# Routing spread over three heads, and five smaller moves, in a fused attention and two-layer mixture-of-experts kernel

## The reference

```python
def _attn_ref(q, k, v):                       # batch 4, 8 heads, 1152 rows, 64 wide
    q_pool = q.reshape(B, H, S // 2, 2, D).mean(axis=3)
    scores = scale * np.matmul(q_pool, k.transpose(0, 1, 3, 2))
    scores = scores - np.max(scores, axis=-1, keepdims=True)
    attn = np.exp(scores)
    attn = attn / (np.sum(attn, axis=-1, keepdims=True) + 1e-09)
    return np.matmul(attn, v).astype(np.float32)
...
x = np.ascontiguousarray(attn_out.transpose(0, 2, 1, 3)).reshape(B * S, H * D)   # 2304 x 512
x = _moe_ref(x=x, **moe_kwargs)     # rows with x @ w_skip > 0: best of 8 experts by x @ w_gate,
                                    # x + gate * relu(x @ w1[e]) @ w2[e]; other rows pass through
return _moe2_ref(x=x, **moe2_kwargs)  # every row: gate * sigmoid(x @ w_output_gate)[e] * relu(x @ w1[e]) @ w2[e]
```

## Time and profile before

| | |
|---|---|
| three timed executions | 1203.83, 1208.31, 1208.90 us (median 1208.31) |
| profiled execution | 1202.06 us, of which the span of the trace is 1200.3 us |
| TensorE busy | 1136.9 us (95% of the span) |
| VectorE busy | 771.9 us (64%) |
| ScalarE busy | 543.3 us (45%) |
| GpSimd busy | 436.1 us (36%) |
| DMA | 132.61 MB, mean 110 GB/s |
| by stage | attention to about 616 us, first expert layer to about 867 us, second to the end |

### The profile page before, as it was taken

The page is one execution under the profiler, slowest core; times in us unless marked ns, Lnnn a source line. Parts: engine busy times, 40 slices in busy tenths (PEclk is TensorE's granted clock), DMA queues, the critical chain, the costliest instruction groups (busy, mean ns, idle before and its releaser), DMA issues.

```text
span 1200.3 us, 22144 instructions
## 1 busy us (share of the span) xinstructions
PE 1136.9 (95%) x7821; PEld 934.8 (78%) x7821; DVE 771.9 (64%) x1710; ACT 543.3 (45%) x945; POOL 436.1 (36%) x335
## 2 busy tenths in 40 slices
PE   7999999999999999999977999999979999999996
PEld 5767767677677776776756999999869999999995
DVE  6667677776787766877462777766745564565551
ACT  3555555555555555555422444544324334334320
POOL 0766666576656775567750000000000000100000
PEclk9999999999999999999988999999979999999999
DMA  5262222232222322222147801454864454151100
GB/s 123 62 208 67 63 70 60 69 93 67 69 61 70 96 73 63 59 69 57 44 173 253 317 27 41 162 199 162 299 216 175 179 183 167 42 178 35 35 18 14
DMA packets 74398, 132.61 MB, mean 110 GB/s; under 512 B 11040, under 2 KB 29472, under 8 KB 74320
## 3 DMA queue, kind: packets, MB, share of 16 engines
q10 hardware_dynamic: 26240, 69.22, 15.7%
q1 hardware_dynamic: 43424, 50.58, 15.6%
q0 software_dynamic: 4656, 11.79, 3.0%
HBM read 106.12 MB, written 19.24 MB: 104 GB/s over the span
## 4 chain that ended last, share of the span: by engine, by line
PE 77%; DVE 16%; DMA 2%; POOL 1%; issue 1%; ACTq 0%; ACT 0%; SPq 0%; POOLq 0%; DVEq 0%
PE PS L723 22%; PE PS L573 8%; PE PS L489 7%; DVE mx L1020 7%; PE PS L556 6%; PE PS L736 6%; PE PS L543 6%; PE PS L737 6%; PE PS L740 6%; PE PS L557 4%; DVE arena_a L994 3%; DVE KA L1003 2%; DVE KA L1000 2%; PE PS L586 1%; PE PS L610 1%
## 5 line engine op out<-in xcount | busy, mean ns | idle before, releaser
L441 POOL TENSOR_TENSOR arena_a<-arena_a,arena_p 128x576 f32<-128x576 f32 x224 | 327.0, 1460 | 143.4 <-ACT arena_p L839 127.7
L1020 DVE TENSOR_REDUCE mx<-PS 128x1 f32<-128x384 f32 (+1 forms) x480 | 249.6, 552 | 156.9 <-PE PS L543 151.4
L723 PE MATMUL PS<-moe,W 128*128 128x128 f32 x2432 | 281.0, 277 | 2.3 <-ACT moe L922 2.3
L723 PEld LDWEIGHTS PS<-moe,W 128*128 128x128 f32 x2432 | 278.1, 193 | 4.7 <-ACT moe L922 2.9
L839 ACT ACTIVATE arena_p<-PS 128x576 f32<-128x576 f32 x288 | 187.6, 652 | 149.9 <-PE PS L557 144.8
L556 PE MATMUL PS<-QHT,KA 128*128 128x288 f32 x576 | 198.6, 348 | 0.5 <-ACT QLT L850 0.5
L543 PE MATMUL PS<-KA,QHT 128*128 128x384 f32 (+1 forms) x480 | 171.8, 359 | 10.3 <-DVE mx L1020 9.6
L1124 DVE TENSOR_TENSOR W2L<-W2R,W2H 128x1024 fp32r<-128x1024 f32 x148 | 175.1, 1245 | 5.0 <-ACT W2H L811 5.0
L557 PE MATMUL PS<-QLT,KB 65*128 65x288 f32 x576 | 169.3, 297 | 0.0
L811 ACT CAST W2H<-W2R 128x1024 fp32r<-128x1024 f32 x148 | 144.3, 1048 | 46.6 <-PE PS L740 41.1
L573 PE MATMUL PS<-arena_p,arena_a 128*64 128x288 f32 x1152 | 160.5, 414 | 1.1 <-issue 1.1
(11 more groups left out here) (173 smaller groups left out, 1211.4 us busy)
## 6 DMA issues: line engine op xcount, KB each, us to landing
W<-in_moe_w ACTq DMA_DIRECT2D x16, 2048.0 KB, 14.4
W2R<-in_moe_w ACTq DMA_DIRECT2D x16, 2048.0 KB
moe<-xs SPq DMA_DIRECT2D x40, 258.0 KB, 4.3
arena_a<-in_k SPq DMA_DIRECT2D x32, 288.0 KB, 2.9
arena_a<-in_v SPq DMA_DIRECT2D x32, 288.0 KB, 2.7
KB<-KA SPq DMA_DIRECT2D x32, 288.0 KB
arena_a<-in_q SPq DMA_DIRECT2D x32, 256.0 KB, 3.2
xs<-padrow SPq DMA_DIRECT2D x8, 258.0 KB, 4.0
```

The costliest lines, as they stand in the source:

```text
L441: nc.gpsimd.tensor_tensor(Acc[u], Acc[u], P[u][:, t, :], ALU.add).then_inc(acc_step, 1)
L723: last = nc.tensor.matmul(PS[:, HB + f // 4, (f % 4) * PN:(f % 4 + 1) * PN], W1[s][:, d, f * PN:(f + 1) * PN], xT[:, d, :], start=(d == 0) ...
L1020: vec.reduce_max(mx3[0:n, t, c:c + 1], PS[0:n, MXB + b % 2, 0:KB_], AX.X).then_inc(pr_max, 1)
```

## The change

Six things are moved; no arithmetic is added or removed.

1. The routing steps of a batch stand in three heads instead of two (`RT_GAPS`); its ranks, exponentials and scatters come one head later.
2. The third of the three block matmuls of t = 4 (`prior` of block 10) stands behind `weighted` and `sums`, no longer ahead of them.
3. `trans_k(g, 1)` waits for the first low part only (`3 * g + 1`).
4. `back_sums` stands behind the last block matmul and directly ahead of `back_logits`, no longer between the two halves of t = 6.
5. The first expert's w2 is split in heads 3 to 6, one chunk each, no longer in head 31. The loads of later weights follow: w2 of expert 2 at the end of head 8, w1 of expert 2 behind the first expert's tiles, and w1 and w2 of expert 10 behind the start of the second layer.
6. In `tile_route` the rank, `Racc` and `Raccb` stand ahead of the wait for `os_free` and the copy to `os_`.

```diff
-        RT_GAPS = {(0, 5): range(4), (0, 10): range(4, 8), (1, 5): range(10, 14), (1, 10): range(14, 18)}
-        SCATTER_IN = {at + 2 + n: (b, range(2 * n, 2 * n + 2)) for b, at in enumerate(RANKS_IN) for n in range(TB // 2)}
+        RT_GAPS = {(0, 5): [0], (0, 10): [1, 2, 3], (0, NBLK): [4, 5], (1, 5): [6], (1, 10): [7], (1, NBLK): [8, 9],
+                   (2, 5): [10, 11], (2, 10): [12, 13, 14, 15], (2, NBLK): [16, 17]}
+        SCATTER_IN = {at + 3 + n: (b, range(2 * n, 2 * n + 2)) for b, at in enumerate(RANKS_IN) for n in range(TB // 2)}
...
+        SPLIT_IN = [3, 4, 5, 6]
...
-                    pe.wait_ge(k_lo, 3 * g + 2)
+                    pe.wait_ge(k_lo, 3 * g + 1)
...
-                    if t == 6 and before:
-                        back_sums(h - 1)
...
                     if t == 4:
-                        if after:
-                            prior(h + 1, next(blocks))
                         if before:
                             weighted(h - 1, 2)
                             sums(h - 1)
+                        if after:
+                            prior(h + 1, next(blocks))
...
-                    if t == 6 and h in RANKS_IN:
-                        ranks_of_batch(RANKS_IN.index(h))
+                    if t == 6 and h - 1 in RANKS_IN:
+                        ranks_of_batch(RANKS_IN.index(h - 1))
                     if t == 6 and before:
+                        back_sums(h - 1)
                         back_logits(h - 1)
...
-                    if h == NH - 1 and 1 <= t <= WCH:
+                    if h in SPLIT_IN and t == 4:
                         act.wait_ge(w2_in[0], 16)
-                        w2_high(0, 0, [t - 1])
+                        w2_high(0, 0, [SPLIT_IN.index(h)])
...
+                if h == SPLIT_IN[-1] + 2:
+                    act.wait_ge(w_lo[0], 1)
+                    load_w2(2)
...
                 if m == 0:
                     act.wait_ge(out_done, NH)
-                    act.wait_ge(w_lo[0], 1)
-                    load_w2(2)
-                    load_w1(2)
+                else:
+                    load_w2(E + 2)
+                    load_w1(E + 2)
...
+                    if w == 0:
+                        load_w1(2)
                     if w + 3 < 2 * E:
                         act.wait_ge(w_lo[m], end + 1)
-                        load_w2(w + 3)
                         act.wait_ge(h_done[m], end * 2)
-                        load_w1(w + 3)
+                        if e < E - 1:
+                            load_w2(w + 3)
+                            load_w1(w + 3)
...
+                    if h in SPLIT_IN and b == 10:
+                        w2_low(0, 0, 0, [SPLIT_IN.index(h)])
+                    route_in(b)
                 if has(h + 1):
                     negate_max(h + 1)
-                if h == NH - 1:
-                    w2_low(0, 0, 0)
                 if has(h - 1):
                     divide(h - 1)
-                if first is not None:
-                    route_step(first, 8)
-                    route_step(first, 9)
+                route_in(NBLK)
...
-                dve.wait_ge(os_free, i + 1)
-                vec.tensor_copy(os_, ob).then_inc(os_done, 1)
                 dve.wait_ge(t_rank, i + 1)
                 then_wait(vec.tensor_tensor(tx[:, :], PS[:, RKB, 0:NR], regbase[:, :], ALU.add))
                 then_wait(vec.tensor_tensor_reduce(out=tx[:, :], in0=tx[:, :], in1=tR[:, :], scale=1.0, scalar=0.0,
                                                    op0=ALU.mult, op1=ALU.add, accum_out=tpf[:, 0:1]))
+                then_wait(vec.tensor_tensor(Racc[:, :], Racc[:, :], tR[:, :], ALU.add))
+                vec.tensor_copy(Raccb[:, :], Racc[:, :]).then_inc(rt_acc, 1)
+                dve.wait_ge(os_free, i + 1)
+                vec.tensor_copy(os_, ob).then_inc(os_done, 1)
                 dve.wait_ge(os_done, i + 1)
                 vec.tensor_tensor(tpu[:, :], tpf[:, :], tinv[:, :], ALU.add).then_inc(t_pos, 1)
-                then_wait(vec.tensor_tensor(Racc[:, :], Racc[:, :], tR[:, :], ALU.add))
-                vec.tensor_copy(Raccb[:, :], Racc[:, :]).then_inc(rt_acc, 1)
```

17 lines of the change are left out of this document (8 added, 9 removed).

## The result

| | before | after |
|---|---|---|
| timed executions, median | 1206.07 us (4 runs, 1201.98 to 1208.90) | 1184.38 us (4 runs, 1183.79 to 1186.12) |
| span of the profiled execution | 1200.3 us | 1182.0 us |
| TensorE busy | 1136.9 us | 1129.2 us |
| VectorE busy | 771.9 us | 759.1 us |

The changed kernel is 1.8% faster: ratio 0.9823, 95% interval 0.9803 to 0.9844. I had predicted 1189 (1178 to 1202).

A forecast was written before the change was run, and what follows sets the result against it. TensorE, busy 95% of the span, was taken as the bound. Terms -9 - 11.2 - 0.4 + 4 - 2.4 - 6.3 - 2.3 + 8 = -19.6 us from 1208.31 gave 1189; range 1178 to 1202, the forecast's own 1182 to 1197.

The forecast's parts named there:

- Ordinary heads: Attention heads: edits 2 and 4 directly save 0.3 us in 30 heads (-9), earlier query pooling 0.40 in 28 (-11.2).
- The earlier pooling: VectorE's query pooling, early in a head: GpSimd's last addition ends about 0.40 us earlier through edit 4, -11.2 over 28 heads.
- The new wait at block 12: After block 10's move, block 12 needs its maximum: late by 0.09 us plus 0.10 for weights not loaded ahead.
- Ninth key tile: Its 0.28 us wait does not come off, as the fifth block waits anyway: 0 in ordinary heads, -0.4 in the first.
- w2's chunks: Heads 3 to 6, behind block 10's maximum: each chunk costs 1.0 us at block 13's matmul, +4 in all.
- Head 31: Split gone from there: value products begin earlier and, no longer the additions, bound the row sums: -2.4 us.
- Loads: Layer starts: row tile arrives early, -6.3 us; loads behind first tile cost 0; second layer's start 0, bound +2.
- Tile routing: Between the layers, edit 6: the count no longer waits for a scatter, net -2.3 us, bounds 0 and -4.
- Routing: Edit 1, routing steps in three heads: 4.0 us per batch against 1.3, so +2.7 each, +8 in all.
- each may wait for an addition: Head ends: steps 4 and 5, likewise 16 and 17, may each wait for GpSimd; next max and pooling some 1.4 us late.

The follow-up runs named there:

- experiment six: Changed kernel with each w1 load one expert later, so two loads, not three, queue behind the first tile and one at the second layer's start: 1183.70 us, ratio 0.9833.
- experiments four: The kernel before with only edits 2 and 4 applied: 1200.37 us, ratio 0.9942.
- seven: Changed kernel with edit 1 alone taken back, routing steps in two heads at their old places: 1199.22 us, ratio 0.9957.

## Why the prediction was right, and where its steps were not

The time came out 4.6 us below the forecast, inside its own range, and the main mechanism, the gain in the ordinary heads, was as I described it. Of the 4.6 us, 2.2 lie in the kernel before: the forecast starts from its median over three runs, 1208.31, and with the fourth run that is 1206.07. That the rest is so small is luck. By the traces the gain is 18.3 us where I had 19.6, but routing cost 7.4 us less than forecast, while the loads (2.6 and 1.6) and the tile routing (3.2) brought 7.4 less.

- **Ordinary heads** (predicted 20.2 us, two terms): 0.65 per head; over 30 heads 19.5. Edit 2 alone is worth 0.45 (predicted 0.17 to 0.3), edit 4 alone 0.32 (predicted 0.40 + 0.10); each is measured with the other in place, and together they make 0.65. The earlier pooling is shown: 0.30 of edit 4's gain stand ahead of the fifth block. The new wait at block 12 is there and in size: 0.16 us of loss where I had 0.19. What I mis-sized is the gain against it, 0.48 behind block 9 where I had 0.36, and I overlooked that edit 2 also makes GpSimd's additions end earlier, for another 0.12 ahead of the fifth block.
- **Ninth key tile** (0): right.
- **w2's chunks** (4.0): 3.3, at block 13 as predicted, right in place and nearly in size. But this is the price of the place that I took as given; it is 0 where block 10 is early, and 0.8 us in all behind block 5. The chunk (VectorE) and the wait (TensorE) of the changed kernel in head 3:

```profile
88.28 1.21 DVE L1131 TENSOR_TENSOR W2L<-W2R,W2H 128x1024 fp32r<-128x1024 f32 x1
```

```profile
90.02 0.39 PE L545 MATMUL PS<-KA,QHT 128*64 128x384 f32 x1 [0.61 <-DVE mx L1027]
```

- **Head 31** (2.4): 2.6, read from the traces and not tried by itself. The additions are still the bound, and not the products as I had it: the last row sums wait 0.22 us for GpSimd (596.42).
- **Loads** (6.3, and 0 for the three behind the first tile): 3.7 net over the first three tiles, 5.4 at the second less 1.7 at the third. The row tile did come early and TensorE waited 1.45 us for VectorE's part where I had 0.8. The 0 was too low: the third load's issue held ScalarE's queue for 4.46 us and TensorE then waited for ScalarE (experiment six). The loads at the second layer's start: a loss of 1.6 (bound 2), though that stretch scatters by as much, and with one load instead of two (experiment six) it was no shorter, 16.82 against 16.77 us.
- **Tile routing** (2.3): wrong. Edit 6 costs 1.5 us in the tile loop and some 0.5 at the last tile, and its gain doesn't exist, since with the loads gone the scatter that it avoids is no longer late. I costed the edit on the trace of before and not on the one that edit 5 leaves. I also overlooked that the copy now stands between the ranks and the tile's output.
- **Routing** (8, or 2.7 more per batch than before): wrong in size, 0.2 more per batch. At a head's end only one step met an addition (203.22 1.37 below), not two, and the pooling behind had to wait for that addition anyway; it ended 1.88 and not 1.77 into the head. The step that failed is "each may wait for an addition; max and pooling of the next head then come some 1.4 late".

VectorE and GpSimd of the changed kernel at the end of the first routing head:

```profile
202.93 0.25 DVE L1082 TENSOR_TENSOR gc<-gc,gcm 96x96 f32<-96x96 f32 x1
203.22 1.37 DVE L1085 TENSOR_TENSOR Rb<-gc,do 96x96 bf16<-96x96 f32 x1
204.51 1.01 DVE L1027 TENSOR_REDUCE mx<-PS 128x1 f32<-128x384 f32 x2
205.44 0.92 DVE L1001 TENSOR_TENSOR arena_a<-arena_a 128x320 f32<-128x320 f32 x1
```

```profile
202.93 3.09 POOL L443 TENSOR_TENSOR arena_a<-arena_a,arena_p 128x576 f32<-128x576 f32 x2 [0.38 <-ACT arena_p L840]
```

What the prediction missed altogether is how much the parts depend on one another. I added a cost for edit 1 and a gain for edit 2. In fact edits 2 and 4 without edit 1 save 0.65 us in each ordinary head, and the six routing heads then cost 15.0 and 16.5 us more than before (experiments four and seven: 1200.37 and 1199.22 us), and only the spread over three heads, with its shorter runs of steps, lets edit 2 pay. Read from the kernel before, edit 1 looks like a loss; with edit 2 it is worth 15 us.

Still open: whether without the third load the 1.7 us at the third tile would come back when the second tile is quick, and what decides whether the clock falls between the layers. I tried no run that holds TensorE busy there.

## What to carry to other kernels

Price each part of a combined change in the schedule that the other parts leave, not in the one of before: here a "cost" was what made the largest gain possible, and a "gain" had been taken by another part. A matmul moved behind a long block opens a gap for its consumer ahead of it and closes the one behind it; work that lived in the old gap has to move too. And where an operation can be blocked by another engine, look for a place in which the block falls into idle time, rather than for one without a block.
